# Scores of the last two of four batches: one fp32 product per three heads, or one stacked fp32r product per head

## What is computed

```
m_new = max(f + m, i);  f_stab = exp(f + m - m_new);  i_stab = exp(i - m_new)
C = f_stab * C + i_stab * outer(v_t, k_t);   n = f_stab * n + i_stab * k_t
y_t = sigmoid(o_t) * (C q_t) / max(|n . q_t|, 1)
x = y with heads side by side: (4, 768, 320)
h = relu(x^T @ w_tok1) @ w_tok2;  u = x + h^T
out = u + relu(u @ w_ch1) @ w_ch2          # d_ch = 1536
```

## Time and profile before

| | |
|---|---|
| median of 3 runs | 459.21 us (458.84 to 459.58) |
| profiled execution | 460.83 us, its span 459.1 us |
| PE matmul busy | 440.7 us, 96% of the span |
| PE weight load busy | 407.9 us, 89% |
| DVE busy | 259.1 us, 56% |
| ACT busy | 209.4 us, 46% |
| POOL busy | 209.1 us, 46% |
| DMA | 47.38 MB, mean 103 GB/s |

### The profile page before, as it was taken

One profiled execution on the slowest core, in us unless ns is written; L12 is line 12 of the kernel. 1 busy time (PEld: TensorE's weight loads), 2 busy tenths in 40 slices (PEclk: granted clock), 3 DMA queues, 4 the chain that ended last, 5 costly groups with the idle time before them and its releaser, 6 DMA issues.

```text
span 459.1 us, 9511 instructions
## 1 busy us (share of the span) xinstructions
PE 440.7 (96%) x3463; PEld 407.9 (89%) x3463; DVE 259.1 (56%) x592; ACT 209.4 (46%) x517; POOL 209.1 (46%) x293
## 2 busy tenths in 40 slices
PE   7899989998999998999999998999999998999996
PEld 3587878998999997999999997899999997999996
DVE  8588965678865346776663236677674326222212
ACT  3665449665555247655552136755552213211120
POOL 7524410888886242988871204698883000000000
PEclk9899999999999999999999999999999999999999
DMA  7666991343344414544344013444410010000101
GB/s 215 191 172 192 348 256 39 104 115 129 95 134 136 140 44 115 148 127 131 127 152 141 1 44 87 144 135 140 126 60 1 1 43 1 0 2 0 45 1 43
DMA packets 36617, 47.38 MB, mean 103 GB/s; under 512 B 3357, under 2 KB 29083, under 8 KB 36571
## 3 DMA queue, kind: packets, MB, share of 16 engines
q1 hardware_dynamic: 35674, 45.76, 33.1%
q10 hardware_dynamic: 896, 1.02, 0.6%
HBM read 42.73 MB, written 4.03 MB: 102 GB/s over the span
## 4 chain that ended last, share of the span: by engine, by line
PE 83%; issue 6%; DVE 4%; ACT 3%; POOL 2%; DMA 1%; ACTq 0%; DVEq 0%; POOLq 0%
PE pC L1151 32%; PE pA L1222 7%; PE pA L1223 7%; PE pA L1224 7%; PE pS L1063 6%; PE pA L1151 5%; PE pY L1120 4%; PE pA L1226 3%; PE pA L1227 3%; PE pY L1099 2%; PE pN L1075 2%; DMA x<-o_gate_dram 1%; PE pA L1181 1%; POOL vw L517 1%; DVE pb L860 1%
## 5 line engine op out<-in xcount | busy, mean ns | idle before, releaser
L974 DVE SCALAR_TENSOR_TENSOR h_lo<-pA,h_hi 128x384 fp32r<-128x384 f32 x96 | 53.5, 557 | 148.0 <-ACT h_hi L755 147.9
L755 ACT ACTIVATE h_hi<-pA 128x384 fp32r<-128x384 f32 x96 | 46.9, 489 | 138.7 <-PE pA L1227 138.6
L1151 PE MATMUL pC<-wc_hi,h_hi 128*128 128x320 f32 x288 | 94.1, 327 | 0.8 <-DVE wc_lo L841 0.8
L1151 PE MATMUL pC<-wc_lo,h_hi 128*128 128x320 f32 x288 | 88.7, 308 | 0.0
L1151 PE MATMUL pC<-wc_hi,h_lo 128*128 128x320 f32 x288 | 88.5, 307 | 0.0
L489 POOL TENSOR_TENSOR gb<-gb,pb 128x384 f32<-128x384 f32 (+1 forms) x54 | 51.7, 957 | 65.7 <-ACT pb L623 65.4
L1222 PE MATMUL pA<-uT_hi,wc_hi 128*128 128x384 f32 x192 | 65.3, 340 | 1.9 <-DVE uT_hi L952 1.9
L1223 PE MATMUL pA<-uT_lo,wc_hi 128*128 128x384 f32 x192 | 64.7, 337 | 0.0
L1224 PE MATMUL pA<-uT_hi,wc_lo 128*128 128x384 f32 x192 | 64.3, 335 | 0.0
L1151 PEld LDWEIGHTS pC<-wc_hi,h_hi 128*128 128x128 f32 x288 | 54.0, 188 | 2.1 <-DVE h_lo L974 1.1
L1151 PEld LDWEIGHTS pC<-wc_lo,h_hi 128*128 128x128 f32 x288 | 54.2, 188 | 0.1
(11 more groups left out here) (128 smaller groups left out, 885.0 us busy)
## 6 DMA issues: line engine op xcount, KB each, us to landing
gb<-g_dram SPq DMA_DIRECT2D x18, 512.0 KB, 4.0
kv<-kvN_dram SPq DMA_DIRECT2D x24, 324.0 KB, 4.1
kd<-kT_dram SPq DMA_DIRECT2D x24, 180.0 KB
qz<-qT_dram SPq DMA_DIRECT2D x72, 60.0 KB
out_dram<-u SPq DMA_DIRECT2D x24, 160.0 KB, 1.9
qd<-qT_dram SPq DMA_DIRECT2D x20, 180.0 KB, 2.6
gq<-g_dram SPq DMA_DIRECT2D x45, 60.0 KB
wc_raw<-w_ch_dram SPq DMA_DIRECT2D x6, 384.0 KB, 5.8
```

What stands on the lines that cost most here:

```text
L755: nc.scalar.activation(h2[0][:, slot % 2], pA[slot % 2][:, 0:HALF], ACT.Relu).then_inc(h2_hi, 1)
L974: nc.vector.scalar_tensor_tensor(h2[1][:, slot % 2], pA[slot % 2][:, 0:HALF], 0.0, h2[0][:, slot % 2].bitcast(F32), ALU.max, ALU.subtract) ...
L1151: ins = mm(dst, a[p], b[q], start=first and n == 0, stop=last and n == 2)
```

## The change

For batches 0 and 1 nothing changes in the scores. For batches 2 and 3 (`HALVED = 2`) keys and queries are cut once into a rounded half (fp32r, by ACT) and a remainder (by DVE), one chunk of one batch at a time, during the steps 5, 8, 11, 14, 17 and 20 of the batch before. Both halves go to a tensor in device memory, `halves`. For each step three loads of 40 partitions stack them in a ring of four buffers, `stack`, on 120 partitions: rounded keys against query remainders, key remainders against rounded queries, rounded against rounded. One fp32r matmul of 128 columns per head then gives that head's scores. `gq` has two buffers in place of three, so that its load waits for the chunk two before. `kd` and `qz` share their room with `stack`. The rest of the diff moves waits and counts to fit, and the host hands over the keys and queries once more in an order by step (`qk`).

```diff
+HALVED = 2
+RING = 4
+HALVES_AT = 5
...
+        halves = nc.dram_tensor("halves", [B - HALVED, NC, ROWS, 4, GH * L], F32, kind="Internal").ap()
...
+        stack = sb("stack", [ROWS, RING, 2, GH * L])
...
+        qk_raw = sb("qk_raw", [ROWS, 2, GH * L])
+        qk_high = sb("qk_high", [ROWS, 2, GH * L], F32R)
...
-        gq = sb("gq", [ROWS, Q, NG, L])
+        gq = sb("gq", [ROWS, R, NG, L])
...
+        def halved(ba, m):
+
+            i, rest = divmod(m - HALVES_AT, NG)
+            return NC * (ba + 1 - HALVED) + i if rest == 0 and 0 <= i < NC and HALVED <= ba + 1 < B else None
...
+            def load_query_decays(ba, c):
+
+                if c > R:
+                    last_ba, last_c = ba, c - R
+                elif ba > 1:
+                    last_ba, last_c = ba - 1, NC - 1 if c % R else NC - R
+                else:
+                    last_ba, last_c = 0, Q + c % R
+                sp.wait_ge(q_scaled, inters(last_ba, last_c))
+                sp.wait_ge(st_added, NG * ((NC - 2) * last_ba + min(last_c, NC - 2)))
...
+            def load_raw(n):
+
+                if n > 0:
+                    sp.wait_ge(halves_out, 16 * HALVES_DMAS * n)
+                sp.dma_start(qk_raw[:, :, :], qk[n // NC, n % NC]).then_inc(raw_in, 16)
+
+            def store_halves(n):
+                row = halves[n // NC, n % NC]
+                sp.wait_ge(halved_hi, n + 1)
+                sp.dma_start(row[:, 3, :], qk_high[:, 0, :].bitcast(F32)).then_inc(halves_out, 16)
+                sp.dma_start(row[:, 0, :], qk_high[:, 1, :].bitcast(F32)).then_inc(halves_out, 16)
+                sp.wait_ge(halved_lo, n + 1)
+                sp.dma_start(row[:, 1:3, :], qk_raw[:, :, :]).then_inc(halves_out, 16)
+
+            def load_step(ba, m):
+
+
+                c, g = divmod(m, NG)
+                k = stacked(ba, m)
+                sp.wait_ge(halves_out, 16 * HALVES_DMAS * (NC * (ba - HALVED) + c + 1))
+                sp.wait_ge(s_mm, STEPS * HALVED + max(k - RING + 1, 0))
+                rows_g = halves[ba - HALVED, c, g * D:(g + 1) * D]
+                for i, pair in enumerate((slice(0, 2), slice(2, 4), slice(0, 4, 3))):
+                    sp.dma_start(stack[i * D:(i + 1) * D, k % RING], rows_g[:, pair, :]).then_inc(stack_in[k % RING], 16)
...
+            def load_chunk(ba, c):
+
+                halving = ba + 1 if HALVED <= ba + 1 < B and c >= R else None
+                first = NC * (ba + 1 - HALVED)
+                load_decays(ba, c)
+                if halving and c > R:
+                    store_halves(first + c - R - 1)
+                if ba < HALVED:
+                    load_scores(ba, c)
+                else:
+                    load_step(ba, NG * c)
+                    load_step(ba, NG * c + 1)
                 load_values(ba, c)
+                if halving:
+                    load_raw(first + c - R)
+                if ba >= HALVED:
+                    load_step(ba, NG * c + 2)
                 if c > 0:
                     load_inter(ba, c)
...
+                n = halved(ba, m)
+                if n is not None:
+                    act.wait_ge(raw_in, 16 * (n + 1))
+                    nc.scalar.activation(qk_high[:, :, :], qk_raw[:, :, :], ACT.Copy).then_inc(halved_hi, 1)
...
+                n = halved(ba, m)
+                if n is not None:
+                    dve.wait_ge(halved_hi, n + 1)
+                    nc.vector.tensor_tensor(qk_raw[:, :, :].bitcast(F32R), qk_raw[:, :, :], qk_high[:, :, :].bitcast(F32),
+                                            ALU.subtract).then_inc(halved_lo, 1)
...
+                if ba >= HALVED:
+                    i = stacked(ba, m)
+                    pe.wait_ge(stack_in[i % RING], 16 * STACK_DMAS * (i // RING + 1))
+                    keys_i, queries_i = [stack[:, i % RING, side, :].bitcast(F32R) for side in range(2)]
+                    for j in range(n):
+                        cols = slice(j * L, (j + 1) * L)
+                        last = mm(scores_bank(ba, m)[:, cols], keys_i[:, cols], queries_i[:, cols], start=True, stop=True)
+                    last.then_inc(s_mm, 1)
+                    return
```

More of the change, by code:

```diff
@@ L179, in program @@
         gb_in = [sem(f"gb_in{i}") for i in range(Q)]
-        gq_in = [sem(f"gq_in{i}") for i in range(Q)]
+        gq_in = [sem(f"gq_in{i}") for i in range(R)]
+        raw_in = sem("raw_in")
+        halved_hi = sem("halved_hi")
+        halved_lo = sem("halved_lo")
+        halves_out = sem("halves_out")
+        stack_in = [sem(f"stack_in{i}") for i in range(RING)]
         g_out = sem("g_out")
@@ L409, in store, with next_batch @@
                     sp.dma_start(out[b, s * L:(s + 1) * L, :], u[:, s, 0:DM]).then_inc(out_done[half], 16)
+            def next_batch(ba):
+                first = NC * (ba - HALVED)
+                load_decays(ba, 0)
+                store_halves(first + 3)
+                load_values(ba, 0)
+                load_raw(first + 4)
+                store(ba - 2, 0)
+                load_decays(ba, 1)
+                store_halves(first + 4)
+                load_raw(first + 5)
+                for m in range(RING):
+                    load_step(ba, m)
+                load_values(ba, 1)
+                load_inter(ba, 1)
+                store_halves(first + 5)
+                store(ba - 2, 1)
+                for m in range(RING, 2 * NG):
+                    load_step(ba, m)
             for b in range(B):
@@ L1057, in step_scores @@
                 n, r = HEADS[g], c % R
[L1058 removed]
+                if g == 0 and ba < HALVED:
                     pe.wait_ge(qk_in[r], 16 * QK_DMAS * (ba * (NC // R) + c // R + 1))
```

97 lines of the change are left out of this document (54 added, 43 removed).

## The result

| | before | after |
|---|---|---|
| median, 4 runs each | 459.39 us (458.84 to 459.85) | 478.04 us (477.42 to 479.28) |
| profiled span | 459.1 us | 476.9 us |

The ratio is 1.041, with a 95% interval of 1.0383 to 1.0437: the change is slower by 4.1%. The forecast was 449.7.

What follows compares the result with a forecast made beforehand. PE was taken as the bound (busy 96%, 83% of the chain of waits). Savings of 11.0 - 0.7 - 0.3 - 0.5 = 9.5 us off 460.8 give 451.3, less 1.6 for profiling: 449.7 us, range 447 to 457.5.

Steps and rivals of the forecast that it cites:

- The price of the product: Score steps of batches 2 and 3: 0.10 us per fp32r product, so 0.30 for three heads and 0.20 for two.
- So time that is taken from PE in a step is gained, until the next engine is full: Middle chunks: PE is never idle, so shorter scores shrink a chunk from 12.57 to 11.65 us; POOL is nearest to full.
- gain of 10.0: Scores of batches 2 and 3: 11.0 us saved, less 0.7 at step 0 and 0.3 at steps 1 and 2.
- this test: Batch 3, which has no loop: the forecast is wrong if it does not gain 4 to 5 us.
- The byte length is the likelier: Batch 2's closed loop from exp(gq) to exp(gq): 12.1 us by bytes at 348 GB/s, against 10.8 by issues.
- the loss of 0.5: Chunks 3 to 5 of batch 2: loop 0.45 over the chunk, 1.35 in all, slack takes 1.2; with engine interference, 0.5 us.
- The landing of `gq`: Last link of batch 2's loop: gq lands 2.6 us after its issue, as qd did.
- the rival that I gave 0.06: The loop runs away: batch 2's gq lands after 8.3 us, loop 17.8, loss 17.3, time 466.5 us; chance 0.06.
- The rival of slow stack loads: Batch 2's 40-partition stack loads run at 215 GB/s: loop 14.0, loss 5.9, time 455.1 us; chance 0.20.
- With the change 211.3. So 1.2 us of slack: Split slots in batches 0 and 1's mixing: DVE ends at 210.1, PE needs it at 211.3, so the split costs PE nothing.
- The sign that the prediction named: Border of batches 0 and 1, last split ahead of x_hi: a PE wait there would show the forecast wrong.
- In batch 1 the chunk stays at 12.6 and the loop is hidden: Batch 1's chunks: they keep their 12.6 us, longer than the loop, so no loss there.

Runs made afterwards that it cites:

- e10: The change with only one of its twelve splits, and DVE's addition into the state put behind the values in batches 2 and 3: 454.50 us, ratio 0.9893.
- e3: The change with 11 of 12 splits left out (raw loads, copies, subtractions, stores); all stack loads read the one split chunk: 460.40 us, ratio 1.0037.
- e14: The kernel before with only DVE's addition into the state put behind the values in batches 2 and 3: 457.62 us, ratio 0.9976.
- e17: As e13, with the stack loads of a batch's steps 4 and 5 issued behind its output gates: 463.97 us, ratio 1.0106.
- e2: The change with ACT's copy of raw keys and queries moved ahead of exp(gb), exp(gq) and vb: 465.73 us, ratio 1.0128.
- e13: The full change with e2's early copy and e10's late addition into the state: 465.05 us, ratio 1.0134.
- e18: As e13, but each stack load after the first four steps brings half of its columns; same issues and waits: 458.90 us, ratio 0.9994.
- e7: The change with all twelve splits and stores but fp32 scores in all batches and no stack loads: 468.69 us, ratio 1.0179.
- e4: The change with one stack load of 120 partitions a step in place of three of 40, same bytes: 474.89 us, ratio 1.0343.
- e12: e13 with two raw buffers by turns in batch 2, three stack buffers in place of four, and loads reordered: 486.01 us, ratio 1.0593.
- e8: As e2, but high halves stored for the first chunk only, 0.37 MB a chunk less written: 464.57 us, ratio 1.0110.

## Why the prediction was wrong

**The price of the product: right.** 0.28 and 0.17 measured for 0.30 and 0.20. A chunk in which nothing else intrudes takes 11.71 (e10) for 11.65.

**"So time that is taken from PE in a step is gained, until the next engine is full": wrong.** It cost the forecast about half of its gain of 10.0: e3, which has the products without the loop, is no faster than the kernel before, and e10 is 5.9 us under e3 by the order of DVE's work, of which the kernel before gains 1.4 too (e14). I read DVE's 8.43 of 12.57 us as room. DVE's work is not even over the steps. In the step with the values it works 4.95 us with no wait named (324.86 to 329.81 in the kernel after), and a step of PE is now 3.9 long. The kernel before showed it already: 4.58 us there, against a step of PE of 4.15. Every third step PE waits, 0.43 us by the trace and 0.66 by the step's length: 4.57 where 4.15 - 0.24 = 3.91 was due. That holds the chunk at 12.35, and batch 3 gained 1.3 us. I named this test myself (batch 3 must gain 4 to 5 us). The early steps of batches 2 and 3 did not gain either. In e10 the stretch from batch 2's step 1 to its step 6 takes 22.54 us for 22.53 before, where the prediction expected more than 1 us from it. In part that is the output gates, whose loads now stand behind two more steps' stack loads: with them ahead, in e17, the stretch takes 21.6.

**"The byte length is the likelier": the right loop, mis-sized.** 12.1 forecast, 16.9 to 17.4 measured. In the sum it was the loss of 0.5; the change is 17.6 us over e3, which leaves the loop out. e2, which takes one link out of the loop, brings 12.3 of them back.
- The wait of the raw load for the stores was left out: 3.9 to 4.3 us. It stands in the order rows (`[waits halves_out]`), and I put the raw load down as an issue of 0.35.
- The landing of `gq`, taken as 2.6 from the earlier trace rows, was 7.7 to 8.4. The 8.3 of the earlier trace rows was the right row, in the rival that I gave 0.06. That rival had the place right and a loop of 17.8, near the measured one partly by luck, since it too left out the wait for the stores and took 348 GB/s for the bytes. Its time of 466.5 is 11.5 us short, because it kept the gain of 10.0.
- The rate, taken as 348 GB/s, was 200. Where the rate is divided by the share that the engines were busy, the middle chunks of batch 2 give 228 / 0.85 = 268 in e13, 223 / 0.83 = 269 in e18, 208 / 0.77 = 270 in e7 and 202 / 0.76 = 266 in the kernel after.

**The sum of bytes that was missing.** I summed the loop's bytes, not the chunk's. By the page's sizes a chunk of batch 2 now moves 512 (gb), 324 (kv), 180 (qd), 180 (gq), 1080 (stack), 360 (raw) and 720 (stores), 3356 KB, or 3.44 MB; before it was 1556 KB. As an estimate, at the 268 GB/s of the line above that is 12.8 us a chunk, more than the forecast's whole chunk of 11.65, with the engines never idle. e18, with 2.88 MB, comes to 10.8 and ran at 12.4 a chunk. e2 and e13 ran at 14.0, and the change at 15.7.

**The rival of slow stack loads.** Its sign in batch 2 was right (chunks longer, ACT idle before `exp(gq)`), and its cause was not. e4 loads the same bytes on 120 partitions at a time and still took 474.9 of 478.0 us, at 205 GB/s with a share of 0.79, or 259. By the rule in the Trainium skill (DMA: Bandwidth & Descriptors, Why a DMA increments its semaphore by 16 and not by 1), loads of 120 rows would use 15 engines where those of 40 use 10. The trace does not bear the rule out as the cause here.

**"With the change 211.3. So 1.2 us of slack": wrong place.** It nearly held for the ordinary steps of e7, where three chunks lost 0.9 us. Where DVE empties `pC` (L1104) lateness reaches PE: 6.3 us of wait in the change, 2.6 in e7. The sign that the prediction named, a wait at the border of batches 0 and 1, did not come: from batch 1's step 17 to batch 2's step 0 it is 18.75 us for 18.68.

**"In batch 1 the chunk stays at 12.6 and the loop is hidden": wrong by a little.** Batch 1 took 2.8 us more. Its step over 106.89 to 113.77 takes 6.88 us where the kernel before takes 5.58. PE is idle in it for 0.96 us, where it was 1.22; it is busy for 5.92 in place of 4.36, at a granted clock of 0.75. The step ahead of it is 0.8 longer and ends with a wait of 0.6 on DVE.

**What was no term at all.** The clock: the second middle chunk has 2.5 us of PE busy time over its neighbour of the same work, at a clock of 0.81. The sum priced waits at their length only.

Open: whether the 1.2 us between 12.8 and the 14.0 of e2 and e13 are the order of the queue, since e12 did not cut the chain cleanly; why e8 gained so little; and what each split costs in batch 1.

## What to carry to other kernels

Before PE's work is shortened, look at the fullest step of each neighbour, not at its share of the chunk: the step that DVE fills sets the pace, and moving out of it something that nobody waits for was worth 5.9 us here, where the shorter products alone were worth nothing. Add up all bytes of a chunk against the rate that crowded stretches show, and take landings from there too. In a loop over one buffer, write down every wait between its links, in particular those of a queue that only seems to issue.
